# The pair products of two levels written in place and copied by ScalarE, with joined VectorE instructions, in a chunked linear-attention and two-expert kernel

## The chip, the cores and the metric

The kernel runs on one core of a Trainium2 chip. The metric is the device time of one execution in microseconds. Engines are named as the profile has them: PE is TensorE's matmuls and PEld its weight loads, DVE is VectorE, ACT is ScalarE, POOL is GpSimd, SP is SyncE, which here issues all transfers.

## The reference

Three parts follow each other, all in float32. The first is a linear attention with a decay per channel, over 4 batches, 8 heads, 768 steps and 48 channels:

```python
for t in range(S):
    cur = einsum('bhd,bhe->bhde', u[None] * kt, vt)
    y[:, :, t] = einsum('bhd,bhde->bhe', rt, state + cur)
    state = wt[:, :, :, None] * state + einsum('bhd,bhe->bhde', kt, vt)
```

Its output, 3072 rows of 384, goes through `x @ w_in` (384 x 2048), an activation (0 below -1, `(h + 1)**2 / 4` between, h above 1) and `@ w_out` (2048 x 384), and then through a second layer of the same sizes with an ELU between the two products.

## The kernel before

**Tiling.** The 768 steps are cut into six chunks k of 128 steps (`CH`). A chunk's 32 batch-heads are two groups g of 16 (two batches each); a group lies as eight columns of heads j on two partition halves a, 64 channels each (48 used). `r_`, `w_`, `k_` hold 8 x 128 columns per group, `a_` holds the attention coefficients of 16 heads, 128 x 128 each, steps s on partitions.

**Levels.** The coefficients are built by seven levels l (`NL`). Level l splits the chunk in blocks of m = 2^l steps: an odd block's queries are multiplied with the keys of the even block before it. TensorE does the products in `pair_products` (L436): for each head 64 x 64 stationary keys times 64 of the queries, once per half h of the keys, 32 matmuls a level; for the last level only one half of the keys counts, so 16 matmuls, all to the lower 64 partitions of the bank. VectorE evicts in `level` (L780): for level 0 a multiplication with a mask (L788), for levels 1 to 5 a copy under a mask (L796), each in two instructions, one for each half of `a_` and its bank. The last level is evicted by ScalarE in `last_level` (L680, two copies of 64 partitions x 512; all of ScalarE's copies stand at L638 in the profile, as all matmuls stand at L434). Then VectorE multiplies the odd blocks of r by the decay of the block before (L808) and the even blocks of k by that of the block behind (L810), and later, in `next_decays` (L818), joins the decays in pairs. Level l + 1 of a group waits for these (`r_updated`, `k_updated`, `decay_ready`). Both groups use the banks `g_bank` (group 1 of chunk 0 uses `down_bank`), so a level's products also wait until those of the level before it in the order, of whichever group, are evicted (`masked`, counted in instructions: two a level).

**After the levels** `turn_k`, `attend`, `state_step` and `turn_x` make a batch's output, the next state and the transposed input of the first layer, with `k_turned_of`, `x_hi_of` on ScalarE and `output`, `next_state`, `x_lo_of` on VectorE.

**Order of the work.** It is written out by hand for each engine, and each works through its own list in order. First comes a startup of 12 slots (`STARTUP`, L586, L757, L946): chunk 0's levels of both groups in turn, then its rows. In it the first layer's weights are split in a high and a low part, in 28 pieces (`W1_PIECES`): the transfer waits until its staging buffer is free (L323), ScalarE casts (`hi_of_weights`), four pieces a slot from slot 1 on, GpSimd subtracts (`lo_of_weights`, L374), and ahead of pieces 12 and 24 GpSimd does `times_keys`, `times_bonus` and `diagonal_output` (L384, L390, L399). The first layer's matmuls wait for all low parts (L601) and for chunk 0's `x_lo`. Then come 6 x 16 slots of the first layer (`layer1_slot`): nine matmuls of 512 columns for `up`, nine for `down` of the slot before the last, three activations on ScalarE, `hi_of_g` and `lo_of_g`. The next chunk's levels are woven in between by `levels_at` (L222): one level in a slot, as a rule between `up` and `down`; in the first 16 slots, which prepare chunk 1, group 1's levels come behind `down`, so that slots 4 to 6 hold two. ScalarE's `last_level` stands at the end of its slot, behind the activations. Then come 6 x 16 slots of the second layer, without attention.

## Time and profile before

| | |
|---|---|
| median of 3 timed runs | 1062.67 us (1061.73 to 1063.42) |
| the profiled execution | 1061.1 us |
| its span in the profile | 1059.0 us |
| PE busy | 1008.0 us, 95% |
| DVE busy | 611.5 us, 58% |
| ACT busy | 494.6 us, 47% |
| POOL busy | 65.8 us, 6% |
| first matmul of the first layer | at 84.67 us |
| second layer | from about 600 us |

An engine's busy share is a mean over stages that have different limits. Matmuls are pipelined: one of 512 columns is on record with some 395 ns, and the next one starts about 230 ns after it, so the pace is read from the starts. Each attention matmul (float32) has two records. A count such as x64 stands for merged records that follow each other.

### The profile page before, as it was taken

What the parts mean: (1) busy time and instruction counts of PE and PEld (TensorE: products, weight loads), DVE (VectorE), ACT (ScalarE), POOL (GpSimd) and SP (SyncE); (2) the same over time, 40 slices, a digit from 0 to 9 for tenths busy, and PEclk for the clock granted to TensorE, in tenths of its full rate; (3) what the DMA queues carried; (4) which work ended last, traced back from release to release, by engine and by line L of the source; (5) the groups of instructions that cost most, each with busy time, mean ns of one, the idle gap of its engine ahead of it and who ended that gap; (6) DMA issues with size and microseconds to landing.
All of it is one profiled execution on the core that took longest, in us unless ns stands there. A gap on an engine that the chain in (4) does not pass through costs nothing.

```text
span 1059.0 us, 23096 instructions
## 1 busy us (share of the span) xinstructions
PE 1008.0 (95%) x10088; PEld 814.5 (77%) x10088; DVE 611.5 (58%) x962; ACT 494.6 (47%) x835; POOL 65.8 (6%) x50
## 2 busy tenths in 40 slices
PE   4377999999999999999999999999999999999998
PEld 3366788777777787878778888888888888888886
DVE  6986967867777777777764364533433334334332
ACT  2223444535354444345444676544454454444443
POOL 6942100000000000000000000000000000000000
PEclk8558999999999999999999999999999999999999
DMA  8415023102203020302022300000000000000000
GB/s 314 125 29 210 3 82 122 39 21 117 76 32 124 13 76 32 136 2 106 2 91 93 117 30 30 1 31 30 30 25 7 30 30 30 4 27 1 31 1 30
DMA packets 24691, 61.70 MB, mean 58 GB/s; under 512 B 2448, under 2 KB 6928, under 8 KB 24592
## 3 DMA queue, kind: packets, MB, share of 16 engines
q1 hardware_dynamic: 24592, 60.24, 15.7%
q8 instruction: 79, 1.29, 0.5%
q14 instruction: 20, 0.16, 0.1%
HBM read 50.79 MB, written 9.44 MB: 57 GB/s over the span
## 4 chain that ended last, share of the span: by engine, by line
PE 91%; DVE 5%; DMA 2%; issue 1%; POOL 1%; SPq 0%; ACT 0%; ACTq 0%; DVEq 0%; POOLq 0%
PE down_bank L434 39%; PE up_bank L434 28%; PE g_bank L434 17%; PE y_bank L434 5%; DMA att<-kT_dram 1%; DVE att L810 1%; DVE att L818 1%; DVE att L808 1%; PE y_bank L475 1%; DVE att L796 1%; PE y_bank L541 1%; SPq L277 0%; POOL ynat L399 0%; POOL wout_lo L374 0%; DMA scratch<-w_out_dram 0%
## 5 line engine op out<-in xcount | busy, mean ns | idle before, releaser
L434 PE MATMUL down_bank<-g_hi,wout_lo 128*128 128x512 f32 x576 | 236.7, 411 | 0.0
L638 ACT CAST g_hi<-scratch 128x512 fp32r<-128x512 f32 x192 | 119.4, 622 | 245.2 <-PE down_bank L434 135.2
L434 PE MATMUL down_bank<-g_hi,wout_hi 128*128 128x512 f32 x576 | 227.5, 395 | 0.0
L434 PE MATMUL down_bank<-g_lo,wout_hi 128*128 128x512 f32 x576 | 227.2, 395 | 0.0
L877 DVE TENSOR_TENSOR g_lo<-scratch,g_hi 128x512 fp32r<-128x512 f32 x192 | 132.7, 691 | 105.1 <-ACT g_hi L638 103.1
L434 PE MATMUL up_bank<-x_hi,win_lo 128*128 128x512 f32 x432 | 174.7, 404 | 2.0 <-DVE x_lo L883 2.0
L434 PE MATMUL up_bank<-x_hi,win_hi 128*128 128x512 f32 x432 | 171.8, 398 | 0.0
L434 PE MATMUL up_bank<-x_lo,win_hi 128*128 128x512 f32 x432 | 171.5, 397 | 0.0
L434 PEld LDWEIGHTS down_bank<-g_hi,wout_lo 128*128 128x128 f32 x576 | 108.5, 188 | 25.6
L434 PEld LDWEIGHTS down_bank<-g_hi,wout_hi 128*128 128x128 f32 x576 | 108.5, 188 | 25.2
L434 PEld LDWEIGHTS down_bank<-g_lo,wout_hi 128*128 128x128 f32 x576 | 108.8, 189 | 21.1
L434 PEld LDWEIGHTS g_bank<-att 64*64 64x64 f32 x4576 | 84.7, 142 | 46.1 <-issue 32.8
L434 PE MATMUL g_bank<-att 64*64 64x64 f32 x4576 | 95.3, 230 | 22.5 <-DVE att L810 13.0
L710 ACT ACTIVATE scratch<-up_bank,consts 128x512 f32<-128x512 f32 x96 | 66.1, 689 | 75.1 <-PE up_bank L434 70.8
L434 PEld LDWEIGHTS up_bank<-x_hi,win_lo 128*128 128x128 f32 x432 | 82.0, 190 | 21.8 <-issue 2.2
L434 PEld LDWEIGHTS up_bank<-x_hi,win_hi 128*128 128x128 f32 x432 | 82.0, 190 | 19.3
L434 PEld LDWEIGHTS up_bank<-x_lo,win_hi 128*128 128x128 f32 x432 | 82.2, 190 | 17.9
L918 DVE SCALAR_TENSOR_TENSOR scratch<-scratch 128x512 f32<-128x512 f32 x96 | 66.0, 688 | 45.4 <-ACT scratch L719 45.4
L796 DVE COPY_PREDICATED att<-masks,g_bank 128x512 f32<-128x512 int32 x110 | 73.4, 720 | 26.8 <-PE g_bank L434 24.7
L936 DVE SCALAR_TENSOR_TENSOR scratch<-scratch,up_bank 128x512 f32<-128x512 f32 x48 | 33.0, 688 | 91.5 <-ACT scratch L741 91.5
L936 DVE SCALAR_TENSOR_TENSOR scratch<-scratch,g_bank 128x512 f32<-128x512 f32 x48 | 33.0, 689 | 85.3 <-ACT scratch L741 85.3
L808 DVE TENSOR_TENSOR att<-att 128x512 f32<-128x512 f32 x84 | 62.2, 740 | 7.3 <-PE g_bank L434 7.2
(83 smaller groups left out, 1128.2 us busy)
## 6 DMA issues: line engine op xcount, KB each, us to landing
att<-rT_dram SPq DMA_DIRECT2D x12, 512.0 KB, 4.0
att<-kT_dram SPq DMA_DIRECT2D x12, 512.0 KB, 5.9
att<-wT_dram SPq DMA_DIRECT2D x12, 512.0 KB, 6.8
r_nat<-rN_dram SPq DMA_DIRECT2D x12, 384.0 KB, 6.8
k_nat<-kN_dram SPq DMA_DIRECT2D x12, 384.0 KB, 8.2
att<-vN_dram SPq DMA_DIRECT2D x12, 384.0 KB, 7.3
x_dram<-r_nat SPq DMA_DIRECT2D x18, 256.0 KB, 2.3
ynat<-x_dram SPq DMA_DIRECT2D x6, 768.0 KB, 4.3
```

The lines of the kernel that those rows point to most:

```text
L434: return nc.tensor.matmul(out, lhsT, rhs, start=start, stop=stop, **kw)
L475: last = nc.tensor.transpose(banks(k, b)[0][:, i * P:(i + 1) * P], k_[g][:, j * CH:(j + 1) * CH], ident[:, :])
L541: last = nc.tensor.transpose(banks(k, b)[3][:, m * P:(m + 1) * P], ynat[:, b, m * P:(m + 1) * P], ident[:, :])
L638: return nc.scalar.copy(out, in_)
L710: nc.scalar.activation(act_buf[f % 2], up_bank[f % 2][:, :], ACT.Relu, bias=consts[:, 0:1], scale=0.5).then_inc(p_ready, 1)
L796: nc.vector.copy_predicated(a[:, half, :].rearrange("p (n two m) -> p n two m", two=2, m=m)[:, :, 1, :], masks[:, l:l + 1, :].broadcast_to ...
L808: nc.vector.tensor_tensor(r[:, :, 1, :], r[:, :, 1, :], w[:, :, 0, 0:1].broadcast_to(shape), ALU.mult).then_inc(r_updated[g], 1)
L810: nc.vector.tensor_tensor(kk[:, :, 0, :], kk[:, :, 0, :], w[:, :, 1, 0:1].broadcast_to(shape), ALU.mult).then_inc(k_updated[g], 1)
L818: nc.vector.tensor_tensor(w[:, :, 0, 0], w[:, :, 0, 0], w[:, :, 1, 0], ALU.mult)\
L877: nc.vector.tensor_tensor(g_lo[:, F % 2, :], act_buf[F % 2], g_hi[:, F % 2, :].bitcast(F32), ALU.subtract).then_inc(glo_ready, 1)
L918: nc.vector.scalar_tensor_tensor(out=act_buf[f % 2], in0=act_buf[f % 2], scalar=1.0, in1=qbuf, op0=ALU.min, op1=ALU.add).then_inc(g_ready, 1)
L936: nc.vector.scalar_tensor_tensor(out=act_buf[f % 2], in0=act_buf[f % 2], scalar=-1.0, in1=up_banks[f % len(up_banks)][:, :], op0=ALU.add, ...
```

## The change

- Level 5: products of 32 keys and 32 queries per block, in place of 64 x 64, written side by side so that no mask is needed; two ScalarE copies in place of two VectorE instructions. There are still 32 matmuls, with 32 stationary columns and 32 moving ones.
- Level 6: odd heads j go to the upper 64 partitions, even ones to the lower. ScalarE copies each half, two instructions as before.
- `last_level` becomes `block_level`, for both. In the startup group 0's level 5 stands in ScalarE's list between pieces 17 and 18, group 1's between 19 and 20.
- Levels 0 to 4 are evicted by one VectorE instruction over both banks (1024 elements) in place of two.
- r and k lie side by side in `att`; their odd and even blocks are multiplied in one instruction (2 x 512 elements) with one semaphore, `rk_updated`. Its size is the same for all levels.
- The counts of `masked` follow (`NMASKED`).

```diff
+NMASKED = [1] * (NL - 2) + [2, 2]
-        r_, w_, k_, v_, a_ = ([a[:, sum(widths[:i]):sum(widths[:i + 1])] for a in att]
+        r_, k_, w_, v_, a_ = ([a[:, sum(widths[:i]):sum(widths[:i + 1])] for a in att]
...
                 for j in range(GP):
                     for a in range(2):
                         ps = slice(a * PAD, (a + 1) * PAD)
...
+                        keys = k_[g][ps, j * CH:(j + 1) * CH]
+                        if l == NL - 1:
+
+                            half = slice((j % 2) * HALF, (j % 2 + 1) * HALF)
+                            out = product_banks(k, g)[half, a, j // 2 * PAD:(j // 2 + 1) * PAD]
+                            last = mm(out, keys[:, 0:HALF], odd_steps(g, l, a, j))
+                            if j >= GP - 2:
+                                last.then_inc(g_filled[g], 1)
+                            continue
+                        if l == NL - 2:
+                            for h in range(2):
+                                out = product_banks(k, g)[h * HALF:h * HALF + m, a, j * m:(j + 1) * m]
+                                last = mm(out, keys[:, h * HALF:h * HALF + m], odd_steps(g, l, a, j)[:, h, :])
...
-            def last_level(k, g):
-
-                act.wait_ge(g_filled[g], k * NFILL + NFILL)
-                for a, products in enumerate(product_banks(k, g)):
-                    later_half = a_[g][0:HALF, a * GP * CH:(a + 1) * GP * CH].rearrange("p (t s) -> p t s", s=2)[:, :, 1]
-                    copy(later_half, products[0:HALF, :]).then_inc(masked[g], 1)
+            def block_level(k, g, l):
+
+                act.wait_ge(g_filled[g], k * NFILL + 4 * l + 4)
+                heads = a_[g].rearrange("p (a j t s) -> p a j t s", a=2, j=GP, s=2)
+                if l == NL - 1:
+                    for parity in range(2):
+                        products = product_banks(k, g)[parity * HALF:(parity + 1) * HALF, :, 0:GP // 2 * PAD]
...
+                m = 2 ** l
+                for h in range(2):
+                    s = slice(h * HALF, h * HALF + m)
+                    products = product_banks(k, g)[s, :, 0:GP * m].rearrange("p a (j t) -> p a j t", t=m)
+                    copy(heads[s, :, :, m:HALF, h], products).then_inc(masked[g], 1)
...
+                if NL - 2 < f <= NL:
+                    block_level(0, 1, f - 1)
                 more_pieces(f)
-                if f == NL - 1:
-                    last_level(0, 0)
+                if NL - 2 <= f < NL:
+                    block_level(0, 0, f)
                 more_pieces(f)
...
-                elif l < NL - 1:
+                elif l < NL - 2:
                     m = 2 * 2 ** l
...
+                    nc.vector.copy_predicated(
+                        a_[g].rearrange("p (n two m) -> p n two m", two=2, m=m)[:, :, 1, :],
+                        masks[:, l:l + 1, :].broadcast_to([P, 2 * GP, HALF]),
+                        products.rearrange("p (n m) -> p n m", m=m)).then_inc(masked[g], 1)
...
+                blocks = NR // (2 * m)
+                rk = bass.AP(r_[g].tensor, r_[g].offset + m, [r_[g].ap[0], [NR - m, 2], [2 * m, blocks], [1, m]])
+                w = bass.AP(w_[g].tensor, w_[g].offset, [w_[g].ap[0], [m, 2], [2 * m, blocks], [0, m]])
+                nc.vector.tensor_tensor(rk, rk, w, ALU.mult).then_inc(rk_updated[g], 1)
```

## Rows read from the trace of the kernel before

**Rows 1.** The page's part 4: chain that ended last, shares by engine

```profile
PE 91%; DVE 5%; DMA 2%; issue 1%; POOL 1%; SPq 0%; ACT 0%; ACTq 0%; DVEq 0%; POOLq 0%
```

**Rows 2.** Windows: stretch, its us, busy (x instructions) by engine, clock, DMA share, GB/s

```profile
100.00:600.00 500.00, 499.79 (x6926) 399.57 (x6927) 360.96 (x621) 232.37 (x404) 3.34 (x2) 1.00 0.19 68
600.00:1059.00 459.00, 454.52 (x1957) 368.57 (x1955) 173.73 (x243) 236.03 (x383) 0.00 (x0) 1.00 0.06 21
0.00:84.67 84.67, 41.35 (x1052) 37.32 (x1053) 69.68 (x88) 22.12 (x41) 55.31 (x44) 0.66 0.46 156
```

**Rows 3.** Timeline of PE: start us, us, engine, line, operation, tiles, count [idle before]

```profile
301.67 1.16 PE L434 MATMUL g_bank<-att 64*64 64x64 f32 x64
302.76 0.50 PE L434 MATMUL down_bank<-g_hi,wout_lo 128*128 128x512 f32 x1
...
307.14 1.15 PE L434 MATMUL g_bank<-att 64*64 64x64 f32 x32
308.22 0.50 PE L434 MATMUL down_bank<-g_hi,wout_lo 128*128 128x512 f32 x1
```

**Rows 4.** Timeline of PEld (weight loads) in the same two fills

```profile
301.67 1.02 PEld L434 LDWEIGHTS g_bank<-att 64*64 64x64 f32 x64 [0.36 <-issue]
...
307.14 1.01 PEld L434 LDWEIGHTS g_bank<-att 64*64 64x64 f32 x32 [0.37 <-issue]
```

**Rows 5.** Timeline of PE in an attend of chunk 1

```profile
147.60 0.35 PE L434 MATMUL y_bank<-state,att 128*64 128x96 f32 x4
147.78 0.40 PE L434 MATMUL y_bank<-att 128*64 128x48 f32 x8
148.00 0.35 PE L434 MATMUL y_bank<-state,att 128*64 128x96 f32 x4
```

**Rows 6.** Timeline of DVE in the startup

```profile
23.07 1.75 DVE L810 TENSOR_TENSOR att<-att 128x512 f32<-128x512 f32 x1
...
26.35 1.30 DVE L796 COPY_PREDICATED att<-masks,g_bank 128x512 f32<-128x512 int32 x2
27.55 0.69 DVE L808 TENSOR_TENSOR att<-att 128x512 f32<-128x512 f32 x1
...
39.25 2.29 DVE L810 TENSOR_TENSOR att<-att 128x512 f32<-128x512 f32 x1
...
45.76 1.47 DVE L810 TENSOR_TENSOR att<-att 128x512 f32<-128x512 f32 x1
```

**Rows 7.** Lines by shape: count | busy us, mean ns of one | idle before

```profile
L898 DVE TENSOR_TENSOR win_lo<-att,win_hi 128x1536 fp32r<-128x1536 f32 x3 | 5.3, 1758 | 2.0 <-ACT win_hi L638 2.0
```

**Rows 8.** Timeline of ACT: startup, and the slot of chunk 1's level 5

```profile
60.61 1.12 ACT L638 COPY att<-g_bank 64x512 f32<-64x512 f32 x2 [9.06 <-PE g_bank L434]
...
72.32 0.51 ACT L638 CAST wout_hi<-scratch 128x384 fp32r<-128x384 f32 x1 [4.02 <-DMA scratch<-w_out_dram]
...
118.88 0.63 ACT L719 ACTIVATE scratch<-scratch 128x512 f32<-128x512 f32 x1
```

**Rows 9.** Timeline of PE: the first up, and a fill in chunk 1

```profile
84.67 0.47 PE L434 MATMUL up_bank<-x_hi,win_lo 128*128 128x512 f32 x1 [2.03 <-DVE x_lo L883]
...
120.99 1.17 PE L434 MATMUL g_bank<-att 64*64 64x64 f32 x64
```

**Rows 10.** Timeline of POOL in the startup

```profile
19.85 4.41 POOL L374 TENSOR_TENSOR win_lo<-scratch,win_hi 128x512 fp32r<-128x512 f32 x3 [1.39 <-ACT win_hi L638]
24.23 5.14 POOL L374 TENSOR_TENSOR win_lo<-ynat,win_hi 128x512 fp32r<-128x512 f32 x3
...
38.73 2.26 POOL L384 TENSOR_TENSOR r_nat<-r_nat,k_nat 128x768 f32<-128x768 f32 x1
...
43.17 3.51 POOL L374 TENSOR_TENSOR wout_lo<-scratch,wout_hi 128x384 fp32r<-128x384 f32 x3
...
62.19 2.85 POOL L374 TENSOR_TENSOR wout_lo<-ynat,wout_hi 128x384 fp32r<-128x384 f32 x2 [7.39 <-ACT wout_hi L638]
...
68.44 3.69 POOL L374 TENSOR_TENSOR wout_lo<-scratch,wout_hi 128x384 fp32r<-128x384 f32 x3
```

More of the change, by code:

```diff
@@ L125, in build @@
         up_bank = [bank(f"up_bank{i}") for i in range(2)]
-        down_bank = [bank(f"down_bank{m}") for m in range(KT)]
-        g_bank = [bank(f"g_bank{i}") for i in range(2)]
+        down_banks = ctx.enter_context(nc.psum_tensor("down_banks", [P, KT, 512], F32))
+        g_banks = ctx.enter_context(nc.psum_tensor("g_banks", [P, 2, 512], F32))
+        down_bank = [down_banks[:, m, :] for m in range(KT)]
+        g_bank = [g_banks[:, i, :] for i in range(2)]
         y_bank = bank("y_bank")
@@ L138, in product_banks @@
         def product_banks(k, g):
-            return down_bank[0:2] if g == 1 and k == 0 else g_bank
+            return down_banks[:, 0:2, :] if g == 1 and k == 0 else g_banks[:, :, :]
         masks_in = sem("masks_in")
@@ L163, in build @@
         masked = [sem(f"masked{g}") for g in range(2)]
-        r_updated = [sem(f"r_updated{g}") for g in range(2)]
-        k_updated = [sem(f"k_updated{g}") for g in range(2)]
+        rk_updated = [sem(f"rk_updated{g}") for g in range(2)]
         decay_ready = [sem(f"decay_ready{g}") for g in range(2)]
@@ L264, in odd_steps @@
             r = r_[g][a * PAD:(a + 1) * PAD, j * CH:(j + 1) * CH]
-            if l == NL - 1:
-                return r[:, HALF:]
+            if l >= NL - 2:
+                return r.rearrange("p (n two m) -> p n two m", two=2, m=2 ** l)[:, :, 1, :]
             return r.rearrange("p (s n two m) -> p s n two m", s=2, two=2, m=2 ** l)[:, :, :, 1, :]
@@ L452, in pair_products @@
                         ps = slice(a * PAD, (a + 1) * PAD)
[L453 to L458 removed]
+                        keys = k_[g][ps, j * CH:(j + 1) * CH]
[10 more added lines that the diff above has]
+                                last = mm(out, keys[:, h * HALF:h * HALF + m], odd_steps(g, l, a, j)[:, h, :])
+                                if j == GP - 1:
+                                    last.then_inc(g_filled[g], 1)
+                            continue
+                        for h in range(2):
+                            out = product_banks(k, g)[h * HALF:(h + 1) * HALF, a, j * PAD:(j + 1) * PAD]
+                            last = mm(out.rearrange("p (n m s) -> p s n m", m=2 ** l, s=2),
+                                      keys[:, h * HALF:(h + 1) * HALF], odd_steps(g, l, a, j))
                             if j == GP - 1:
[L460 removed]
+                                last.then_inc(g_filled[g], 1)
             def turn_k(k, b):
                 g = b // 2
[L465 removed]
+                pe.wait_ge(rk_updated[g], k * NL + NL)
                 if k == 0:
@@ L678, in k_turned_of @@
                 copy(k_turned[:, (b % 2) * HP * P:(b % 2 + 1) * HP * P], banks(k, b)[0][:, :]).then_inc(kt_copied, 1)
-            def last_level(k, g):
-                act.wait_ge(g_filled[g], k * NFILL + NFILL)
-                for a, products in enumerate(product_banks(k, g)):
-                    later_half = a_[g][0:HALF, a * GP * CH:(a + 1) * GP * CH].rearrange("p (t s) -> p t s", s=2)[:, :, 1]
-                    copy(later_half, products[0:HALF, :]).then_inc(masked[g], 1)
+            def block_level(k, g, l):
[4 more added lines that the diff above has]
+                        products = product_banks(k, g)[parity * HALF:(parity + 1) * HALF, :, 0:GP // 2 * PAD]
+                        copy(heads[0:HALF, :, parity::2, :, 1], products.rearrange("p a (j t) -> p a j t", t=PAD))                            .then_inc(masked[g], 1)
+                    return
+                m = 2 ** l
+                for h in range(2):
+                    s = slice(h * HALF, h * HALF + m)
+                    products = product_banks(k, g)[s, :, 0:GP * m].rearrange("p a (j t) -> p a j t", t=m)
+                    copy(heads[s, :, :, m:HALF, h], products).then_inc(masked[g], 1)
             def tile_out_of_psum(c):
@@ L722, in layer1_slot @@
                 for k, g, l in now + late:
-                    if l == NL - 1:
-                        last_level(k, g)
+                    if l >= NL - 2:
+                        block_level(k, g, l)
                 if c == NC - 1:
@@ L978, in level_masks @@
     parts = []
-    for m in 2 ** np.arange(NL - 1):
+    for m in 2 ** np.arange(NL - 2):
         mask = (s // m % 2 == 0) & (t // m == s // m + 1)
```

57 lines of the change are left out of this document (17 added, 40 removed).

## Prediction

> **What bounds the kernel now.** I first read the chain that ended last, by engine [rows 1]: it is TensorE for 91% and VectorE for 5%. That is an average over stages, so the windows come next [rows 2]. From 100 to 600 us (the first expert layer, with the levels of the next chunk woven in) TensorE is busy for 499.79 of 500 us; VectorE has 361 and ScalarE 232 of the same 500. There, only less work on TensorE shortens the run. From 600 us on (the second layer) the change touches nothing. Before 84.67 us (the startup: chunk 0 alone, and the first layer's weights split by ScalarE and GpSimd) TensorE has work for half of the time and VectorE is busy for 69.68 us. So there are two sums: TensorE's work in `pair_products` behind the startup, and the chain through VectorE, GpSimd and ScalarE in the startup.
>
> **TensorE, level 6 (`l == NL - 1`).** The levels are seen as fills of `g_bank` [rows 3]. A fill of levels 0 to 5 has 64 records (32 matmuls, each recorded twice), starts at 301.67 and is followed by `down` at 302.76: 1.09 us. The fill of level 6 has only 32 records and takes 308.22 - 307.14 = 1.08 us. The first goes round four quadrants of the array (two row halves `a`, two column halves `h`), the second round two. The weight loads give the pace [rows 4]: 64 within 1.02 us, less some 0.14 for the last one, is 14 ns each; 32 within 1.01 is 28 ns each. About 0.2 us of a fill is then fixed: 1.09 - 64 x 0.014. The change sends level 6's heads alternately to the upper and lower partitions, four quadrants again: 32 x 0.014 + 0.2 = 0.64 us, 0.44 less. Ten of the twelve fills lie behind the startup (k = 1 to 5, two groups): **-4.4 us**. A rule speaks against it. The Trainium skill ("TensorE: Matmul & The Clock Gate", Part 1) says that start-to-start never drops below about 25 ns; by that level 6 would save about 0.1 us a fill, 1 us in all, and the forecast would end 3.4 us higher. The 14 ns of [rows 4] contradict it for this very kind of fill, so I give it no chance of its own.
>
> **TensorE, level 5 (`l == NL - 2`).** It keeps 64 records, but each multiplies a 64 by 32 stationary block by 32 columns in place of 64 by 64. No row shows that shape; the nearest show what columns do [rows 5], all with 64 stationary columns in two quadrants: eight records of 48 columns take 148.00 - 147.78 = 0.22 us (27.5 ns each), four of 96 columns 147.78 - 147.60 = 0.18 us (45 ns). That is 0.37 ns a column, so 32 columns would be 28 - 12 = 16 ns in two quadrants, 8 in four. Against that, 48 columns are hardly faster than 64 (27.5 and 28 ns). So a fill lies between 64 x 0.008 + 0.2 = 0.71 and 1.09 us. I take the middle, 11 ns and 0.90 us, as both rows are equally near: 0.19 less, ten times **-1.9 us** (0 to -3.8). It could also be dearer, which is the last rival.
>
> **VectorE, behind the startup.** Joined evictions and joined multiplications move the same elements with fewer instructions. The pace is in [rows 6]: two evictions take 27.55 - 26.35 = 1.20 us, so one of 512 elements follows the next after 0.60, with 0.69 on record. An instruction of 1536 elements has 1.759 us on record [rows 7], so 1024 elements more cost 1.07 and 512 cost 0.535; about 0.07 us of the 0.60 is fixed (an estimate from these rows). Each join saves 0.07 us, to 1.13 for 1024 elements, and level 5's eviction 1.2 us. All this is beside a TensorE that is busy for 499.79 of 500 us [rows 2]: worth nothing there, except for the 0.2 us that TensorE does idle: **-0.2 us**.
>
> **ScalarE, behind the startup.** It gains two copies per level 5. [rows 8] has two such copies, of 64 x 512, at 1.12 us. ScalarE is in order, so they stand ahead of the next `hi_of_g`, and the next fill of the same `g_bank` waits for them. The tightest place is chunk 1, slot 5, where a fill of group 1 follows a fill of group 0 by one `down` only [rows 9]: ScalarE ends its Square at 118.88 + 0.63 = 119.5, the copies would end at 120.6, and TensorE wants the bank at 120.99. Elsewhere a whole slot of about 5.5 us lies between [rows 3]. I cost this at nothing; the cover is 0.4 us once, and if it is gone it costs less than 1 us.
>
> **The startup.** Here VectorE is on the path, and what lengthens it is GpSimd. In [rows 6] the multiplication L810 takes 1.75 us from 23.07, and L808 only 0.69 at 27.55. The difference (some 1.07 us) is one GpSimd instruction: a VectorE instruction with two SBUF inputs and a GpSimd one run alternately, and GpSimd's of 512 columns take 5.14/3 = 1.71 us each beside them [rows 10]. The evictions, from PSUM, don't wait. Per level step VectorE meets this up to three times (r, k, decays); the join makes it two. It removes L810's wait: 1.07 us three times, 1.6 at the 768-wide GpSimd pair (38.73 to 43.17 us; L810 has 2.29 there), 0.8 twice beside the 384-wide pieces (1.47), 6.4 us; plus seven steps by 0.13 for the joins, 0.9; plus level 5's evictions, 2.4. VectorE's chain to level 6 thus ends about 9.7 us earlier.
>
> What is late next is in [rows 8, 10]. GpSimd runs without a break until 54.8, then idles 7.39 us until 62.19, since ScalarE stood in `last_level(0, 0)` until TensorE's level 6 came (9.06 us of idle, to 60.61) and the weight pieces 22 and 23 queue behind it. From 62.19 the chain is GpSimd: two pieces, two `diagonal_output`, the first of three pieces (68.44), its staging buffer's DMA, ScalarE's cast of piece 27 at 72.32, and then `k_turned_of(0, 1)` and all that leads to the first `up` at 84.67 [rows 9]. So the startup can gain at most GpSimd's idle time, 7.4 us, and less by what GpSimd loses. It loses: the joined multiplication holds it for 1.13 us where two of 0.60 took turns with it. In a step of 3.4 us it gets two instructions (1.73 each) against 18.9 us for twelve before (19.85 to 38.73, 1.58 each): +1.9. Then its ten 384-wide pieces, 11.6 us before (43.17 to 54.80), meet the four multiplications of levels 5 and 6, which used to fall into its idle time: 10 x 1.0 + 4 x 0.95 + 0.2 = 14.0, +2.4; the pair between loses nothing worth counting, and I deduct 0.4 for waits of level 4 that have moved forward. 1.9 + 2.4 - 0.4 = 3.9; 7.4 - 3.9 = **-3.5 us**. What follows is shifted as it is: chunk 1's loads wait for the states, so they move with it. ScalarE's new place for level 5 (ahead of pieces 18 and 20) is hidden: TensorE's level 5 then comes near 47 us, when GpSimd by this pace is only at piece 12 or 13. Bounds: -7.4 (GpSimd loses nothing), and a loss of 3 us if each of its 22 pieces is held up by a 1.13 where it met 0.60 (22 x 0.53 = 11.7, 4.3 more than its idle time; the evictions, which don't hold it up, cover one of them).
>
> **Sum.** -4.4 - 1.9 - 0.2 - 3.5 = -10.0. The profiled execution took 1061.1 us (span 1059.0) and the median of the timed runs is 1062.67, so 1.6 more: 1051.1 there, 1052.7 as median.
>
> **Rivals and chances.**
> *Forecast* (GpSimd becomes the startup's bound, narrow fills a bit cheaper): 1052.7, range of its own 1049 to 1056; 0.42.
> *Narrow fills cost the same*, the 14 ns a floor: 1062.67 - 4.4 - 0.2 - 3.5 = 1054.6; 0.20. For it: 48 and 64 columns pace alike [rows 5]; against: 96 don't. The Trainium skill ("TensorEngine Tiling (Array Packing)", Instruction Overhead) has the rule behind it: one column takes as long as sixty, and a tiling factor isn't to be taken from a dimension already small. No row here has fewer than 48 columns.
> *GpSimd keeps its pace* and the startup gets all 7.4 us: this is so if the joined eviction is a little longer than a GpSimd instruction and its gap (1.13 against about 1.22 us), so that GpSimd slips in a second one each step. 1048.8, with the narrow fills at their best 1046.9; 0.18.
> *The startup gives nothing or loses up to 3*: 1056 to 1059; 0.10. *Narrow tiles overlap in two quadrants only*: a fill of 64 x 0.022 + 0.2 = 1.6 us, +0.5 x 10, so 1062.67 - 8.1 + 5 = 1059.6 or, at 28 ns, 1063.5; 0.05, about no change.
> *Slower: the 32-wide tiles don't overlap at all.* 64 x 0.044 + 0.2 = 3.0 us a fill against 1.09, +19 us in ten; 1062.67 - 8.1 + 19 = 1073.6. It decides from a fill of 1.9 us on, where the other gains (8.1/10 each) are spent. Only that the shape isn't in the trace speaks for it; 0.05.
>
> About 0.2% (2.1 us) is what a measurement of this kernel can tell from no change. Faster 0.90, same 0.05, slower 0.05. The range, 1045 to 1060, takes in both bounds of the startup and of the narrow fills.
>
> **What will show it.** Fills of 32 records at 0.64 us and of level 5 between 0.7 and 1.1; TensorE busy without a break from 100 us and its first `up` at about 81 us; multiplications of 1024 elements at 1.2 to 2.3 us in the startup; GpSimd's idle time near 55 us gone or short, and its pieces at about 1.75 us. The prediction is wrong if GpSimd still idles there (the startup gained more), if level 5's fill exceeds 1.1 us, or if TensorE gets new idle time before a fill, waiting for ScalarE's copies.

## The result, and the profile after

The changed kernel takes 1052.89 us (median, 1052.35 to 1053.73); on the same chip the kernel before took 1062.34 (1061.73 to 1063.42). The ratio is 0.9911, with a 95% interval of 0.9894 to 0.9928: 9.45 us faster. Forecast were 1052.7 us and 1045 to 1060. The profiled execution took 1053.15 us, its span 1051.4.

The page of the kernel after, busy time by engine and the shares of the chain that ended last (line in place of [rows 1]):

```profile
PE 1000.0 (95%) x10088; PEld 802.0 (76%) x10088; DVE 581.5 (55%) x794; ACT 509.9 (48%) x859; POOL 69.5 (7%) x50
...
PE 91%; POOL 4%; DMA 2%; SPq 1%; ACT 1%; DVE 1%; issue 0%; ACTq 0%; DVEq 0%; POOLq 0%
```

VectorE had 5% of the chain and GpSimd 1%; now it is 1% and 4%. Nearly everything outside TensorE's 91% is the startup, and its bound has changed owners. The chain itself, in order of time (start us, us, what), shows it more plainly: from 19.55 to about 66 us its long pieces are all GpSimd's, and then a transfer into a staging buffer and the loads of k (`kT_dram`) follow (only the longest pieces of the chain are listed in this view).

```profile
19.55 22.58 POOL win_lo L380 x12
44.01 2.67 POOL r_nat L396
46.69 11.75 POOL wout_lo L380 x9
59.25 2.91 POOL wout_lo L380 x3
62.24 2.90 POOL ynat L405 x2
66.48 2.35 DMA scratch<-w_out_dram
80.42 8.85 DMA att<-kT_dram
```

The windows after (stretch, its us, busy and count by engine in the order PE, PEld, DVE, ACT, POOL, clock, DMA share, GB/s; the first answers to [rows 2]):

```profile
100.00:600.00 500.00, 499.38 (x6902) 397.23 (x6901) 344.99 (x487) 250.01 (x432) 3.34 (x2) 1.00 0.19 68
600.00:1000.00 400.00, 400.00 (x1715) 321.64 (x1714) 154.54 (x218) 208.77 (x340) 0.00 (x0) 1.00 0.06 22
```

TensorE is still the bound from 100 us on, but idles 0.6 us there where it idled 0.2. VectorE has 16 us less of those 500, ScalarE 18 more. What TensorE waits for in that stretch (line, awaited instruction: us in total, times, longest), two waits that the kernel before did not have; the one of 0.21 us that it had, a fill behind VectorE's eviction, is gone:

```profile
PE y_bank L440 <- DVE ynat L878: 0.3, 1, 0.3
PE g_banks L440 <- ACT att L658: 0.2, 1, 0.2
```

TensorE's timeline in slots 4 to 6 of chunk 1 (start us, us, engine, line, operation, tiles, count, idle time before) has both new fills; it answers to [rows 3, 9]:

```profile
115.93 0.76 PE L440 MATMUL g_banks<-att 64*32 64x32 f32 x64
116.62 0.50 PE L440 MATMUL down_banks<-g_hi,wout_lo 128*128 128x512 f32 x1
...
119.09 1.17 PE L440 MATMUL g_banks<-att 64*64 64x64 f32 x64
120.19 0.50 PE L440 MATMUL up_bank<-x_hi,win_lo 128*128 128x512 f32 x1
...
122.48 0.69 PE L440 MATMUL g_banks<-att 64*64 64x64 f32 x32
123.10 0.50 PE L440 MATMUL down_banks<-g_hi,wout_lo 128*128 128x512 f32 x1
```

From fill to the next matmul, level 5 takes 116.62 - 115.93 = 0.69 us and level 6 123.10 - 122.48 = 0.62, where both took 1.09. A fill of levels 0 to 4 is unchanged: 120.19 - 119.09 = 1.10.

The startup after, GpSimd (its only idle time from 19.55 us on, until its last piece, is the one in the last row; answers to [rows 10]):

```profile
19.55 5.40 POOL L380 TENSOR_TENSOR win_lo<-scratch,win_hi 128x512 fp32r<-128x512 f32 x3 [1.37 <-ACT win_hi L658]
24.91 6.23 POOL L380 TENSOR_TENSOR win_lo<-ynat,win_hi 128x512 fp32r<-128x512 f32 x3
...
62.24 2.90 POOL L405 TENSOR_TENSOR ynat<-att,diagonal 128x768 f32<-128x768 f32 x2
65.11 3.20 POOL L380 TENSOR_TENSOR wout_lo<-scratch,wout_hi 128x384 fp32r<-128x384 f32 x3
69.44 1.00 POOL L380 TENSOR_TENSOR wout_lo<-scratch,wout_hi 128x384 fp32r<-128x384 f32 x1 [1.14 <-ACT wout_hi L658]
```

ScalarE's cast of piece 27 (72.32 us in [rows 8]), and TensorE's first `up` (84.67 in [rows 9]) with its first wait in chunk 1:

```profile
68.86 0.51 ACT L658 CAST wout_hi<-scratch 128x384 fp32r<-128x384 f32 x1 [6.48 <-DMA scratch<-w_out_dram]
```

```profile
81.62 0.47 PE L440 MATMUL up_bank<-x_hi,win_lo 128*128 128x512 f32 x1 [2.03 <-DVE x_lo L905]
...
89.31 1.99 PE L440 MATMUL g_banks<-att 64*64 64x64 f32 x64 [4.24 <-DMA att<-kT_dram]
```

**Where the time went.** TensorE's starts cut the span into four parts: to the first `up`; from there to the `up` of slot 3, from where on TensorE alone is the bound (at 103.19 us before, at 101.50 after); on to slot 80, behind the last level; and the rest, nearly all second layer, which nothing of the change touches. Differences to the kernel before, in us, for two profiled executions of the same changed kernel:

| part | before | after | after, a second execution |
|---|---|---|---|
| to the first `up` | 84.67 | -3.05 | -2.73 |
| first `up` to slot 3 | 18.52 | +1.36 | +0.20 |
| slot 3 to slot 80 | 478.55 | -7.99 | -7.96 |
| slot 80 to the last `up` | 464.25 | +2.08 | +0.51 |
| span | 1059.0 | -7.6 | -10.0 |

The third row is the same to 0.03 us in both. The second and the fourth differ by 1.2 and 1.6 us between two executions of one kernel, so they are no property of the change; a comparison of two single profiles is no better than 2 to 3 us here, and the timed medians (-9.45) carry the verdict.

### The profile page after: what moved, and what is told of

Read it like the earlier page. It is cut to its first block, busy times and chain, and to the rows that moved or that the text cites. A ratio compares the mean times of both kernels' runs of the same rounds, so it can differ in the third digit from the quotient of the medians.

```text
span 1051.4 us, 22880 instructions
## 1 busy us (share of the span) xinstructions
PE 1000.0 (95%) x10088; PEld 802.0 (76%) x10088; DVE 581.5 (55%) x794; ACT 509.9 (48%) x859; POOL 69.5 (7%) x50
## 4 chain that ended last, share of the span: by engine, by line
PE 91%; POOL 4%; DMA 2%; SPq 1%; ACT 1%; DVE 1%; issue 0%; ACTq 0%; DVEq 0%; POOLq 0%
PE down_banks L440 39%; PE up_bank L440 29%; PE g_banks L440 16%; PE y_bank L440 5%; POOL win_lo L380 2%; POOL wout_lo L380 2%; PE y_bank L495 1%; DMA scratch<-w_in_dram 1%; DMA att<-kT_dram 1%; SPq L283 1%; PE y_bank L561 1%; POOL ynat L405 0%; POOL r_nat L396 0%; DMA scratch<-w_out_dram 0%; DVE att L834 0%
## 5 line engine op out<-in xcount | busy, mean ns | idle before, releaser
L440 PE MATMUL down_banks<-g_hi,wout_lo 128*128 128x512 f32 x576 | 237.0, 411 | 0.0
L440 PE MATMUL down_banks<-g_hi,wout_hi 128*128 128x512 f32 x576 | 227.8, 396 | 0.0
L440 PE MATMUL down_banks<-g_lo,wout_hi 128*128 128x512 f32 x576 | 226.8, 394 | 0.0
L440 PEld LDWEIGHTS down_banks<-g_hi,wout_lo 128*128 128x128 f32 x576 | 108.2, 188 | 26.3
L440 PEld LDWEIGHTS down_banks<-g_hi,wout_hi 128*128 128x128 f32 x576 | 108.1, 188 | 26.3
L440 PEld LDWEIGHTS down_banks<-g_lo,wout_hi 128*128 128x128 f32 x576 | 108.4, 188 | 21.7
L834 DVE TENSOR_TENSOR att<-att 128x1024 f32<-128x1024 f32 x84 | 104.9, 1248 | 14.4 <-PE g_banks L440 13.9
L440 PEld LDWEIGHTS g_banks<-att 64*64 64x64 f32 (+1 forms) x4576 | 75.1, 138 | 44.2 <-issue 21.7
L440 PE MATMUL g_banks<-att 64*64 64x64 f32 (+1 forms) x4576 | 85.6, 226 | 20.5 <-DVE att L834 10.2
L821 DVE COPY_PREDICATED att<-masks,g_banks 128x1024 f32<-128x1024 int32 x44 | 57.2, 1301 | 23.1 <-PE g_banks L440 21.0
```

Of the source, the lines that this page charges most:

```text
L440: return nc.tensor.matmul(out, lhsT, rhs, start=start, stop=stop, **kw)
L821: nc.vector.copy_predicated(a_[g].rearrange("p (n two m) -> p n two m", two=2, m=m)[:, :, 1, :], masks[:, l:l + 1, :].broadcast_to([P, 2 * ...
L834: nc.vector.tensor_tensor(rk, rk, w, ALU.mult).then_inc(rk_updated[g], 1)
```

## Experiments

Medians of timed runs (the two rows "again" are single executions), ratio to the kernel before on the same chip, and what the one profiled execution of each shows (us). "Startup" is the start of the first `up`, "levels" the part from slot 3 to slot 80, "GpSimd, 12" the time from the start of the first 512-wide piece to the end of the twelfth.

| kernel | median | ratio (95%) | startup | levels | GpSimd, 12 |
|---|---|---|---|---|---|
| before | 1062.34 | 1 | 84.67 | 478.55 | 18.9 |
| before, again | 1061.14 | - | 84.48 | 478.54 | 19.5 |
| after | 1052.89 | 0.9911 (0.9894-0.9928) | 81.62 | 470.56 | 22.6 |
| after, again | 1051.1 | - | 81.94 | 470.59 | 26.6 |
| level 6 alone | 1057.13 | 0.9961 (0.9946-0.9976) | 84.71 | 474.05 | 19.1 |
| level 5 alone | 1054.2 | 0.9933 (0.992-0.9946) | 81.36 | 474.59 | 18.9 |
| joins alone | 1059.52 | 0.9979 (0.9969-0.9988) | 80.91 | 478.63 | 22.4 |
| levels 5 and 6, no joins | 1052.0 | 0.9901 (0.9881-0.992) | 81.43 | 470.24 | 19.1 |
| after, r and k apart | 1051.86 | 0.9909 (0.9896-0.9923) | 82.11 | 470.20 | 26.6 |
| after, 4 pieces to VectorE | 1045.69 | 0.985 (0.9835-0.9866) | 77.31 | 470.41 | 25.7 |
| after, 8 pieces to VectorE | 1045.78 | 0.9854 (0.9838-0.987) | 78.06 | 470.43 | 26.5 |
| after, less GpSimd work | 1046.63 | 0.9859 (0.9846-0.9873) | 78.06 | 470.66 | 22.3 |
| after, 64 keys x 32 queries | 1055.56 | 0.9948 (0.9933-0.9963) | 82.22 | 474.09 | 22.6 |
| after, 32 keys x 64 queries | 1053.29 | 0.9925 (0.991-0.994) | 80.98 | 473.95 | 21.7 |

The profiled executions differ in TensorE's granted clock too: from 20 to 60 us it was 0.50 to 0.54 in most of them, but 1.00 in those of level 5 alone, the joins alone, four pieces to VectorE and both kernels with one narrow dimension. The timed runs show no gain from it: of 42 of the kernel before, the 12 with a mean clock of 0.98 or more over the whole run have a median of 1062.5 us, the 30 others one of 1061.4. In the column "startup" it stays mixed in with the edits.

### Level 6 in four quadrants, alone

```diff
+                            if l == NL - 1:
+                                hs = slice((j % 2) * HALF, (j % 2 + 1) * HALF)
+                                out = product_banks(k, g)[a][hs, j // 2 * PAD:(j // 2 + 1) * PAD]
```

> Level 6 alone goes round four quadrants (ScalarE copies by halves of heads), all else as before. Fills of 32 records take 0.63 us against 1.08: 10 x 0.45 = 4.5 us. In the startup the fill of group 0 at the half clock is some 0.9 us shorter, and it stands on the chain ScalarE, GpSimd; so 5.4 us less in all, 1057. Rival: the startup doesn't move, 4.5 less, 1058. If the pace were a floor per record (25 ns), only 1 us.

Measured: 1057.13 against 1061.49 us, -4.4. All of it lies in the stretch of the levels: 478.55 - 474.05 = 4.50 us, ten steps of 0.45. The small gain expected in the startup did not come (first `up` at 84.71). GpSimd's idle time before pieces 22 and 23 shrank from 7.39 to 6.77 us, but a wait for VectorE's sums of the diagonal took its place. Timeline of POOL in this kernel:

```profile
61.61 2.68 POOL L376 TENSOR_TENSOR wout_lo<-ynat,wout_hi 128x384 fp32r<-128x384 f32 x2 [6.77 <-ACT wout_hi L643]
...
67.16 1.85 POOL L401 TENSOR_TENSOR ynat<-att,diagonal 128x768 f32<-128x768 f32 x1 [0.99 <-DVE diagonal L833]
```

The term of level 6 (-4.4) is right, and the edit changes nothing in the size of the products, only how many quadrants they go round.

### Level 5 narrow and on ScalarE, alone

Edit: the changed kernel with level 6, the evictions and the multiplications put back as before; this is what it keeps.

```diff
+                        if l == NL - 2:
+                            for h in range(2):
+                                out = product_banks(k, g)[h * HALF:h * HALF + m, a, j * m:(j + 1) * m]
+                                last = mm(out, keys[:, h * HALF:h * HALF + m], odd_steps(g, l, a, j)[:, h, :])
```

> Level 5 alone is written 32 wide and copied by ScalarE; level 6, evictions and multiplications are as before. Fills of 64 narrow records take 0.69 us against 1.09: 10 x 0.40 = 4.0 us. Startup: VectorE loses 2.4 us of evictions, but ScalarE now waits for level 5 ahead of pieces 18 to 21; worked through from the rows of before, GpSimd's piece 24 ends near 67.9 us against 69.86, 2 us less. In all 6 us, 1056.3. Rival: ScalarE's new place starves GpSimd, and the startup gives nothing: 4.0 less, 1058.3, or the startup is longer.

Measured: 1054.2 us, -7.3: 3.96 us in the levels (478.55 - 474.59) and 3.31 in the startup. The first is as expected for this run (4.0) and twice the 1.9 of the prediction, as a narrow fill takes 0.69 us and not 0.90; the second is 1.3 more than expected. For the startup, ScalarE's and GpSimd's rows in this kernel:

```profile
52.69 1.24 ACT L657 COPY att<-g_banks 32x512 f32<-32x512 f32 x2 [11.12 <-PE g_banks L440]
```

```profile
54.55 3.59 POOL L380 TENSOR_TENSOR wout_lo<-scratch,wout_hi 128x384 fp32r<-128x384 f32 x3 [4.69 <-ACT wout_hi L657]
...
65.43 1.86 POOL L405 TENSOR_TENSOR ynat<-att,diagonal 128x768 f32<-128x768 f32 x1 [1.58 <-DVE diagonal L849]
```

Without the joins, ScalarE stands in `block_level(0, 0, 5)` for 11.12 us. GpSimd idles 4.69 us there in place of 7.39 later, and VectorE, free of level 5's evictions, is earlier at all that follows.

### The joins, alone

Edit: the changed kernel with levels 5 and 6 put back: one eviction over both banks for levels 0 to 5, r and k in one multiplication.

```diff
-NMASKED = [1] * (NL - 2) + [2, 2]
+NMASKED = [1] * (NL - 1) + [2]
```

> Only the joins: one eviction and one multiplication in place of two each; levels 5 and 6 filled and evicted as before. TensorE's work is as before, so nothing behind the startup. Theory (GpSimd sets the startup's end): VectorE's chain is 7.3 us shorter, but GpSimd's pieces get slower beside 1.13 us multiplications, and the startup ends 3.5 us earlier, 1058.8. Rival (VectorE sets it): 7.3 us earlier, 1055. Rival (GpSimd was the bound already before): nothing.

Measured: 1059.52 us, -2.0. In the profile the first `up` comes 3.76 us earlier, as expected, and GpSimd's idle time is gone; its twelve pieces take 22.4 us in place of 18.9. The levels gain nothing (478.63 against 478.55): the wait of 0.21 us behind VectorE's eviction is gone, and a new one of 0.3 us has come. TensorE's waits from 100 to 600 us in this kernel:

```profile
PE y_bank L440 <- DVE ynat L877: 0.3, 1, 0.3
```

It is the first of the two waits in the changed kernel: at the end of slot 5 of the fifth stretch of 16, `state_step` finds its bank not yet evicted. It stands in six of the eight executions with both joins and in none of the six others, so it goes with the joins, though not in every kernel that has them. Timed, the joins gave 1.8 us less than their startup. 0.3 is this wait; in the profiled execution another 1.07 was in the second layer (465.32 against 464.25), which the joins don't touch.

### Both kernels again, for the spread between executions

> The kernel before once more, for its trace. Behind the startup the trace after gains 0.40 us at each level 5 and 0.45 at each level 6, 9.67 us in all at 553 us of before, but the span is only 7.6 us shorter: in the second layer, which the change doesn't touch, TensorE started 432.5 matmuls in 100 us before and 430.3 after. Theory A: this is a difference between executions (or chips), and the kernel before will show such paces too, so the two profiled spans don't compare to better than 2 us. Theory B: it is a cost of the change (the banks are now two larger tensors); then before shows 432 to 433 again.

> The changed kernel once more, for its trace: what its first up (81.62 us), its wait for chunk 1's k (4.24 us of idle) and its pace in the second layer (430.3 matmuls in 100 us) are in another execution. If these are of the execution and not of the kernel, the wait for k lies anywhere between 2.5 and 4.5 us and the pace between 430 and 433.

Measured: the kernel before agrees with itself (span 1059.0 both times, first `up` 84.67 and 84.48). The changed one does not: 1051.4 and 1049.0. Its startup ran quite differently, and reached its first `up` within 0.32 us of the same time. Timeline of DVE, POOL and PE in the second execution of the changed kernel:

```profile
21.02 1.25 DVE L834 TENSOR_TENSOR att<-att 128x1024 f32<-128x1024 f32 x1
22.14 0.66 DVE L840 TENSOR_TENSOR att<-att 128x256 f32<-128x256 f32 x1
```

```profile
19.73 7.02 POOL L380 TENSOR_TENSOR win_lo<-scratch,win_hi 128x512 fp32r<-128x512 f32 x3 [1.52 <-ACT win_hi L658]
26.72 7.77 POOL L380 TENSOR_TENSOR win_lo<-ynat,win_hi 128x512 fp32r<-128x512 f32 x3
```

```profile
50.55 1.13 PE L440 MATMUL g_banks<-att 64*64 64x64 f32 x32 [11.25 <-ACT att L658]
```

and of DVE in the first:

```profile
20.98 1.22 DVE L834 TENSOR_TENSOR att<-att 128x1024 f32<-128x1024 f32 x1
22.11 1.69 DVE L840 TENSOR_TENSOR att<-att 128x256 f32<-128x256 f32 x1
```

The same multiplication of 256 elements takes 1.69 us in the one and 0.66 in the other: VectorE waits for GpSimd in the first, and in the second GpSimd waits for VectorE (7.77/3 = 2.59 us a piece). The VectorE that never waits is through its levels early, and then TensorE's level 6 stands 11.25 us for ScalarE, whose pieces hang on GpSimd. So the turn-taking decides who waits in the middle, while, by this reading, the sum of GpSimd's work decides when the startup ends. The kernels with less work for GpSimd test that.

### r and k multiplied apart

```diff
-                nc.vector.tensor_tensor(rk, rk, w, ALU.mult).then_inc(rk_updated[g], 1)
+                nc.vector.tensor_tensor(rk[0], rk[0], w[0], ALU.mult)
+                nc.vector.tensor_tensor(rk[1], rk[1], w[1], ALU.mult).then_inc(rk_updated[g], 1)
```

> The changed kernel with r and k multiplied in two instructions of 512 again (evictions still joined, levels 5 and 6 as changed). Theory (VectorE and GpSimd take turns, and GpSimd now sets the startup's end): GpSimd gets three instructions in a step again and its first twelve pieces take about 19 us against 22.6; VectorE's chain gets some 6 us longer, back onto the path. The two nearly cancel: startup -1 to +2 us against the changed kernel, 1052 to 1055. Rival (the join is what made VectorE fast and VectorE is what counts): the startup is 6 us longer, 1059.

Measured: 1051.86 us, ratio 0.9909 where the changed kernel has 0.9911: no difference. But the twelve pieces did not go back to some 19 us; they took 26.6. Timeline of DVE and POOL, one step of VectorE:

```profile
26.96 0.68 DVE L834 TENSOR_TENSOR att<-att 128x512 f32<-128x512 f32 x1
26.97 2.73 POOL L380 TENSOR_TENSOR win_lo<-ynat,win_hi 128x512 fp32r<-128x512 f32 x1
27.56 0.68 DVE L835 TENSOR_TENSOR att<-att 128x512 f32<-128x512 f32 x1
28.16 0.39 DVE L841 TENSOR_TENSOR att<-att 128x128 f32<-128x128 f32 x1
```

The piece takes 2.73 us where the shortest takes 1.26: it stands some 1.5 us, for all three multiplications, and then runs beside the eviction, which starts at 28.46. The second execution of the changed kernel shows the same with the joined multiplication (a piece of 2.64 us from 26.72). In the first execution GpSimd gets in twice a step: a piece that meets the joined multiplication takes 2.37 us (from 20.96), the next one, beside the decays and the eviction, 1.66. Counted from eviction to eviction, GpSimd does three pieces in a step of 5.1 us before the change, two in steps of 3.7 to 3.9 us in the first execution after it, and one in steps of 2.6 to 2.9 us in the second execution and in this kernel.

This kernel's one profiled execution is of the last kind. It shows that multiplying apart does not by itself give GpSimd its three turns back, but not what the joined multiplication costs where GpSimd gets in twice. The last column of the table parts by the eviction: 18.9 to 19.5 us in all five executions with two evictions a level, 21.7 to 26.6 in all nine with the joined one. Only this one execution separates the two joins, and why GpSimd gets three turns, two or one is open.

### Four weight pieces given to VectorE

Pieces 24 to 27 are the last and VectorE is idle there (5.33 and 5.61 us in the changed kernel). They are subtracted by VectorE, around its first output of slot 7.

```diff
-                lo_of_weights(i)
+                if i < NPOOL:
+                    lo_of_weights(i)
...
+                if f == NL:
+                    for i in range(NPOOL, len(W1_PIECES)):
+                        if i == len(W1_PIECES) - 1:
+                            output(0, 0)
+                        dve.wait_ge(w1_hi_ready, i + 1)
+                        nc.vector.tensor_tensor(piece(W1_PIECES[i], False), staged(i),
+                                                piece(W1_PIECES[i], True).bitcast(F32),
+                                                ALU.subtract).then_inc(w1_lo_dve, 1)
```

> The changed kernel with the low parts of the last four weight pieces (24 to 27) on VectorE, behind its last level, where it idles for 5.3 us, in place of GpSimd. If GpSimd sets the end of the startup, piece 27's transfer can start near 61.5 us in place of 66.4 and the first up comes 4 to 5 us earlier, at about 77 us: 1048.5. Rival (VectorE, or the rows of chunk 0, set it): nothing, or slower by VectorE's 4 x 0.5 us.

Measured: 1045.69 us, ratio 0.985: 16.1 us faster than the kernel before on the same chip, and the fastest of all. The first `up` comes at 77.31, 4.3 us before that of the changed kernel (81.62). Timeline of ACT in this kernel, piece 27:

```profile
65.46 0.51 ACT L665 CAST wout_hi<-scratch 128x384 fp32r<-128x384 f32 x1 [0.79 <-DMA scratch<-w_out_dram]
```

Piece 27 is cast 3.40 us earlier than at 68.86, in the changed kernel. So GpSimd's list held the end of the startup in the changed kernel.

### Less work for GpSimd

GpSimd's two 768-wide products of group 1 are left out; two copies of one column stand in their place, ahead of the first piece, where they take 1.7 us together.

```diff
-                if i == 3 * PER_SLOT:
-                    times_keys(0, 1)
-                    times_bonus(0, 1)
```

> The changed kernel without GpSimd's two products for group 1 of chunk 0 (r times k, times u; 4.5 us of GpSimd at 42 to 46.7 us; that part of the output is then left out of the computation). If GpSimd sets the startup's end, it ends about 4.5 us earlier, less 1 us of more contention: 1049.4. Rival (VectorE sets it): VectorE loses two waits of at most 1.6 us at that place, 1 us or less earlier.

Measured: 1046.63 us, and the first `up` at 78.06, 3.56 us earlier than in the changed kernel, for 4.5 us of work taken off the middle of the list (42.09 to 46.65 us there). The run before it says the same: 3.6 to 4.3 us come back at the end, whether GpSimd instructions go from the middle of the list or from its end.

### Eight pieces given to VectorE

```diff
-NPOOL = 24
+NPOOL = 20
```

(against the kernel with four; the `diagonal_output` pair now waits for VectorE's count too)

> The changed kernel with the low parts of the last eight weight pieces (20 to 27) on VectorE, behind its last level. With four moved the first up came at 77.31 us and GpSimd still worked without a break to 64 us. If GpSimd still sets the end of the startup, four more of its pieces away (1.0 us each, less VectorE's 0.5 us each) bring the first up to about 75 us: 1043.5. Rival: ScalarE's list or the rows of chunk 0 set it now, or the four pieces come later than GpSimd would have done them, since VectorE waits for its last level first: 77 us or later, 1045.7 or more.

Measured: 1045.78 us, no better than with four; first `up` at 78.06. GpSimd's last pieces are no longer the bound. Timelines of POOL and ACT, and two pieces of the chain that ended last:

```profile
61.85 3.22 POOL L410 TENSOR_TENSOR ynat<-att,diagonal 128x768 f32<-128x768 f32 x2 [3.30 <-issue]
```

```profile
66.21 0.51 ACT L666 CAST wout_hi<-scratch 128x384 fp32r<-128x384 f32 x1 [2.07 <-DMA scratch<-w_out_dram]
```

```profile
59.84 0.48 DVE wout_lo L994
...
60.39 3.21 DMA scratch<-w_out_dram
```

GpSimd idles 3.30 us and piece 27 is cast no earlier (66.21 against 65.46). The chain still goes through GpSimd's first twelve pieces, but leaves it at 51.85 us; from 57.6 on it is VectorE's last multiplications of chunk 0's levels, its first subtraction, and the transfers into the staging buffers. TensorE's fill of level 6 waited 11.28 us for ScalarE in this kernel.

### The narrow fill: is it the keys or the queries?

Two kernels shrink one dimension only. 64 keys by 32 queries:

```diff
-                                last = mm(out, keys[:, h * HALF:h * HALF + m], odd_steps(g, l, a, j)[:, h, :])
+                                last = mm(out, keys[:, h * HALF:(h + 1) * HALF], odd_steps(g, l, a, j)[:, h, :])
```

> The changed kernel, but level 5 multiplies 64 stationary keys (as before) by 32 moving queries; the other half of the products is not read. The narrow fill took 0.69 us against 1.09 for 64 by 64; I had put it at 0.90 since I only had rows on moving columns. If the moving columns alone set the pace, this fill stays at 0.69. If loading and multiplying follow each other in a quadrant, it lies halfway, near 0.9, and the kernel is 10 x 0.2 = 2 us slower than the changed one. If only the loading counts, 1.09 and 4 us.

and 32 keys by 64 queries:

```diff
-                                last = mm(out, keys[:, h * HALF:h * HALF + m], odd_steps(g, l, a, j)[:, h, :])
+                                last = mm(out, keys[:, h * HALF:h * HALF + m], odd_steps(g, l, a, j))
```

> The changed kernel, but level 5 multiplies 32 stationary keys by 64 moving queries. Moving columns alone: 1.09 us a fill, 4 us slower than the changed kernel. One after the other: near 0.9 us, 2 us slower. Loading alone: 0.69 and nothing.

Measured: neither keeps the gain. Timeline of PE, 64 keys by 32 queries:

```profile
115.96 1.14 PE L440 MATMUL g_banks<-att 64*64 64x32 f32 x64
117.03 0.50 PE L440 MATMUL down_banks<-g_hi,wout_lo 128*128 128x512 f32 x1
```

and 32 keys by 64 queries:

```profile
114.01 1.10 PE L440 MATMUL g_banks<-att 64*32 64x64 f32 x64
115.03 0.50 PE L440 MATMUL down_banks<-g_hi,wout_lo 128*128 128x512 f32 x1
```

A fill takes 1.07 and 1.02 us. With 64 by 64 it is 1.09, with 32 by 32 it is 0.69. So it goes neither by the queries alone nor by the keys alone, nor by their sum: it goes nearly by the larger of the two, and both must shrink. In the stretch of the levels each costs some 3.5 us against the changed kernel (474.09 and 473.95 against 470.56), ten steps of 0.35.

### Levels 5 and 6 without the joins

```diff
-NMASKED = [1] * (NL - 2) + [2, 2]
+NMASKED = [2] * NL
...
+                    for x in range(2):
+                        nc.vector.copy_predicated(
```

(and the same for level 0's multiplication and for r and k)

> Levels 5 and 6 as changed, but no joins: two evictions a level on VectorE and r and k multiplied apart. The joins alone ended the startup 3.7 us earlier (first up 80.91), level 5 alone 3.2 (81.36), all together no more than 2.5 to 3 (81.62, 81.94). If all run into the same bound, GpSimd's list, then without the joins the first up stays within 1 us of 81.5, TensorE's 8.5 us behind the startup stay, and the kernel lies at 1050.5 to 1052, like the changed one. Rival: the joins carry a gain of their own in the whole change; then the first up comes at 84 us or later and the kernel is 2 to 3 us slower than the changed one.

Measured: 1052.0 us, ratio 0.9901 (0.9881 to 0.992), beside the 0.9911 (0.9894 to 0.9928) of the whole change: no difference. First `up` at 81.43, 0.19 us earlier than with the joins. The joins are worth nothing on top of the rest. They reach the same point by another way. Timeline of POOL in this kernel:

```profile
54.33 3.60 POOL L380 TENSOR_TENSOR wout_lo<-scratch,wout_hi 128x384 fp32r<-128x384 f32 x3 [4.28 <-ACT wout_hi L658]
...
65.19 1.85 POOL L405 TENSOR_TENSOR ynat<-att,diagonal 128x768 f32<-128x768 f32 x1 [1.58 <-DVE diagonal L850]
...
67.65 3.25 POOL L380 TENSOR_TENSOR wout_lo<-scratch,wout_hi 128x384 fp32r<-128x384 f32 x3 [0.61 <-ACT wout_hi L658]
```

Here GpSimd idles (4.28, 1.58, 0.61 us) but works faster, and the startup hangs on VectorE's and ScalarE's lists; with the joins GpSimd never idles and works slower.

## Why the prediction was right, and where it was not

**Level 6, -4.4: right.** -4.50 alone, not the 1 us that the prediction set against it and ruled out. The fill went from 1.09 to 0.62 us (0.64 forecast). In four quadrants 32 records pace as 64 do, at 13 to 14 ns.

**Level 5, -1.9: the mis-sized term.** In the stretch of the levels it is -3.96 alone; a step gains 0.40, and the fill takes 0.69 us, not 0.90. The prediction took the middle between a price by columns (0.71) and no gain (1.09). Its price by columns came from [rows 5], where 48 and 96 columns both meet 64 stationary ones, and it noted that 48 pace like 64 without an explanation. The two kernels with one narrow dimension supply it: with 64 stationary columns 32 moving ones pace nearly like 64 (1.07 us), and so 48 columns against 64 stationary ones told nothing of 32 by 32.

The rival "narrow fills cost the same" fell for the fill of this change, and its reason held for half a change: with one dimension at 64, a fill costs 1.07 or 1.02 of 1.09 us. The Trainium skill ("TensorEngine Tiling (Array Packing)", Instruction Overhead) says that one column takes as long as sixty. The traces agree where 64 columns are stationary (1.07 us for 32 moving columns, 1.09 for 64), and disagree where 32 are (0.69 and 1.02 us); no run here has fewer than 32. The rivals "two quadrants only" and "don't overlap at all" would have given fills of 1.6 and 3.0 us; there is nothing of them.

**VectorE's 0.2 us of TensorE's idle time: wrong sign, small.** The 0.21 us that were meant, a fill behind VectorE's eviction, did go. But TensorE now idles 0.6 us in 100 to 600 where it idled 0.2: 0.3 behind VectorE once, which no step had, and twice behind ScalarE's copies, which the prediction had named as a sign of being wrong. The place that it named (chunk 1, slot 5) is one. ScalarE's row in the changed kernel:

```profile
117.72 1.23 ACT L658 COPY att<-g_banks 32x512 f32<-32x512 f32 x2
```

The copies end at 118.95 us and the fill starts at 119.09; TensorE would have wanted it at 118.91 (116.62 and the 2.29 of a `down`). The cover of 0.4 us was used up by the fill of level 5 itself, which is 0.40 shorter and stands just ahead; it costs 0.18 us, too little for the view of waits to name. The wait of 0.2 us that the view names is one slot later, behind the copies of level 6, where the prediction did not look:

```profile
124.26 1.26 ACT L658 COPY att<-g_banks 64x512 f32<-64x512 f32 x2
...
125.66 1.16 PE L440 MATMUL g_banks<-att 64*64 64x64 f32 x64 [0.20 <-ACT att L658]
```

Both together are within the "less than 1 us". In all, 10 x (0.40 + 0.45) less 0.4 us more of idle time is 8.1 us; 7.99 were measured where 4.4 + 1.9 + 0.2 = 6.5 were forecast.

**The startup, -3.5: mechanism right in the main, amount a little high.** GpSimd's 7.39 us of idle time went, GpSimd became the chain, and the first `up` came at 81.62 and 81.94 us in place of 84.67 and 84.48: 2.5 to 3.1 less, and 1.7 to 2.6 less at the `up` of slot 3, as the wait for the loads of k (2.58, 2.88 us before; 4.24, 2.82 after) varies by execution. Within that, one step failed. The loss of GpSimd on its first twelve pieces was put at 1.9 us, from two pieces in a step of 3.4 us, and was 3.7 and 7.7 (22.6 and 26.6 against 18.9). In the first execution the two pieces a step came true, but the step took 3.7 to 3.9 us; the second execution, one piece a step, was not foreseen. The prediction laid the loss to the joined multiplication; the one execution with it taken apart was no faster, and all executions with slower pieces share the joined eviction. The loss on the ten 384-wide pieces (+2.4, to 14.0 us) was about right in the first execution (13.6) and nothing in the second (11.6 as before). The two losses together, 5.7 and 7.7 us, are more than the forecast's 3.9. What made up for them no step had: from the start of piece 22 to the end of piece 24 GpSimd took 6.2 us in both executions in place of 7.7 (VectorE was busy for 2.6 us of the first execution's 6.2 and all through the 7.7), it began 0.3 and 0.1 us earlier, and in the second execution the pair between the pieces took 3.6 us in place of 4.4. So piece 24, whose staging buffer the chain waits for, ended 3.5 and 2.2 us earlier. That this is the forecast's 3.5 in the first execution is luck: two errors that cancel. The rival "GpSimd keeps its pace" fell: in none of the nine executions with joined evictions did it.

The prediction also gave the joins too much weight. It credited them with 6.4 + 0.9 us of VectorE's chain against 2.4 for level 5's evictions; measured, joins or level 5 alone give the same (first `up` at 80.91 and 81.36), and together no more (81.62). Added up, the three parts alone give 4.4 + 7.3 + 2.0 = 13.7 us of the medians, the whole 9.45: the startup's part is paid once only.

**The total.** -10.0 forecast, -9.45 measured. That it is so near is partly luck, by compensation: the levels gave 1.5 us more than forecast, the startup 0.4 to 1.0 less at its first `up` and 0.9 to 1.8 less at slot 3. The rest of the difference between single executions (0.5 to 2.1 us in the second layer) isn't the change's.

## What to carry to other kernels

Where small matmuls stand in quadrants of the array, count first how many quadrants are in use: the same products cost half the time a record when four take turns in place of two (13 ns for 28). Shrinking one dimension of a quadrant's matmul from 64 to 32 gave 0.02 to 0.07 us of 1.09, both together 0.40; an edit that narrows only one is not worth its eviction's trouble. Before joining VectorE instructions beside a GpSimd that shares the stretch, ask who ends it: here GpSimd's total did, so the joins were worth nothing on top of the rest, while moving four of its 28 subtractions to an idle VectorE gave some 6.5 us more ((0.9911 - 0.985) x 1062).

## What the runs showed of the hardware

**The pace in a quadrant.** For 64 records in four quadrants: 64 by 64 in 1.09 us, 64 stationary by 32 moving in 1.07, 32 by 64 in 1.02, 32 by 32 in 0.69. Less the 0.2 us that the prediction read as fixed, that is 14, 14, 13 and 8 ns a record.

**VectorE and GpSimd take turns, and who waits varies by execution.** The Trainium skill ("SBUF — State Buffer", SBUF: two separate sides) has the rule: a VectorE instruction with two SBUF inputs and a GpSimd one exclude each other for a whole instruction. The trace agrees (0.66 or 1.69 us for the same 256 elements). What was not expected is that the same program lets VectorE through every time in one execution and makes it wait once a level in another, with GpSimd's twelve pieces at 26.6 or 22.6 us: one piece a step, or two. With two evictions a level there were three a step, and it stayed at 18.9 to 19.5. The eviction, which reads PSUM and a mask, does not hold a piece up: one of 1.45 us (19.55 to 21.00) runs beside an eviction from 19.78 to 21.09.

**The second layer's pace.** At a granted clock of 1.00 in both, a slot of the untouched second layer took 4.18 us in some executions (464.25 for the stretch in both of the kernel before) and 4.20 in another (466.33 in the changed kernel; 464.76 in its second execution), for 111 slots. The other profiled executions lie at 464.25 to 466.33. In the windows from 600 to 1000 us, x1724 records of PE stand in the kernel before and x1715 in the changed one. It is of the execution and not of the kernel; its cause is open.

**Why the version with four pieces on VectorE gained more than its first `up`** is partly open too. Its first `up` is 4.3 us earlier than the changed kernel's, and by the ratios it is 6.5 us faster (0.985 against 0.9911, intervals of about 0.0016 to either side). Its profiled execution had the second layer at 464.28, not 466.33, and waited 2.76 us for k, not 4.24; that accounts for these two profiles, not for the medians.
